# A fused attention, router and expert kernel: key ranges copied on chip, keys and values loaded one head pair ahead, shorter first loads, other unread matmuls

## What is computed

```python
scores_l = scale * np.matmul(q, k.transpose(0, 1, 3, 2))      # kept where |i - j| < 16
scores_s = scale * np.einsum('bhsd,bhnd->bhsn', q, k_sum) + np.log(block)
a = softmax(concat([scores_l, scores_s]))
out = a @ concat([v, v_sum])
```

## Time and profile before

| | us |
|---|---|
| median of 3 runs | 525.67 |
| lowest, highest | 524.82, 528.15 |
| the profiled execution, its own time | 525.85 |
| its span in the profile | 524.1 |
| around the span | 1.8 |
| mean granted TensorE clock, share of full | 0.952 |

### The profile page before, as it was taken

How to read it: one execution, slowest core, us unless ns; L and a number is a source line. 1 busy time by engine, 2 the same in 40 slices (tenths; PEclk the granted TensorE clock), 3 DMA queues, 4 the chain that set the end, 5 groups by cost and what they waited for, 6 DMA issues and landing times.

```text
span 524.1 us, 8451 instructions
## 1 busy us (share of the span) xinstructions
PE 455.3 (87%) x2824; PEld 402.3 (77%) x2824; DVE 354.3 (68%) x1121; ACT 162.0 (31%) x422; POOL 126.0 (24%) x159
## 2 busy tenths in 40 slices
PE   2899899982039998999999999999999999999992
PEld 0688787871037997987997997899897789899771
DVE  3767697778979789889869968976976530300340
ACT  1678576741010113133322212321410341231230
POOL 3111466992012031032112103112101313010011
PEclk9999999996557998999999999999999999999997
DMA  9989997220008045055017007204402709000001
GB/s 252 274 228 282 301 263 231 68 61 1 0 13 339 0 159 194 0 181 191 21 71 281 21 1 271 102 21 176 175 22 93 280 17 329 28 20 1 0 22 40
DMA packets 30883, 65.89 MB, mean 126 GB/s; under 512 B 6784, under 2 KB 19328, under 8 KB 26752
## 3 DMA queue, kind: packets, MB, share of 16 engines
q0 software_dynamic: 6592, 39.85, 20.7%
q1 hardware_dynamic: 23680, 24.57, 16.9%
q10 hardware_dynamic: 576, 1.02, 0.6%
HBM read 59.14 MB, written 6.29 MB: 125 GB/s over the span
## 4 chain that ended last, share of the span: by engine, by line
PE 74%; DVE 12%; ACT 3%; DMA 3%; issue 3%; SPq 3%; POOL 0%; DVEq 0%; ACTq 0%; POOLq 0%
PE psum L906 16%; PE psum L923 15%; PE psum L966 5%; PE psum L973 4%; PE psum L967 4%; PE psum L943 4%; PE psum L944 4%; PE psum L948 4%; DVE key_wide L1205 3%; PE psum L750 3%; DMA shared<-vT 3%; PE psum L775 2%; PE psum L997 2%; PE psum L853 2%; PE psum L759 2%
## 5 line engine op out<-in xcount | busy, mean ns | idle before, releaser
L1205 DVE TENSOR_SCALAR_CACHE_REDUCE key_wide<-keys,thr 128x1536 bf16<-128x1536 f32 x49 | 88.6, 1809 | 1.0
L906 PE MATMUL psum<-shared,w_sb 128*128 128x192 f32 x512 | 86.1, 330 | 1.3 <-ACT shared L662 1.3
L923 PE MATMUL psum<-xs,w_sb 128*128 128x192 f32 x512 | 87.0, 328 | 0.0
L906 PEld LDWEIGHTS psum<-shared,w_sb 128*128 128x128 f32 x512 | 84.9, 193 | 2.0 <-issue 1.5
L923 PEld LDWEIGHTS psum<-xs,w_sb 128*128 128x128 f32 x512 | 83.0, 190 | 0.0
L552 POOL DMA_INDIRECT w_sb<-w,widx x32 | 31.2, 974 | 153.8 <-DVE widx L1276 112.9
L750 PE MATMUL psum<-w_sb,shared 128*128 128x376 f32 x96 | 42.5, 527 | 10.9 <-DMA w_sb<-k_win 10.2
L1304 DVE TENSOR_TENSOR yT_lo<-psum,yT_hi 128x384 fp32r<-128x384 f32 x16 | 8.9, 556 | 55.7 <-ACT yT_hi L662 55.7
L625 ACT ACTIVATE keys<-keys,nmax 128x184 f32<-128x184 f32 x96 | 41.8, 438 | 12.9 <-DVE nmax L1089 12.5
L1089 DVE CUSTOM_DVE_ANT_0 keys<-psum,w_sb 128x184 f32<-128x184 f32 x96 | 29.7, 346 | 22.6 <-PE psum L750 19.7
L966 PE MATMUL psum<-wout_hi,turned_hi 128*128 128x512 f32 x96 | 38.5, 401 | 4.2 <-ACT turned_hi L662 4.2
(11 more groups left out here) (145 smaller groups left out, 817.3 us busy)
## 6 DMA issues: line engine op xcount, KB each, us to landing
w_sb<-k_win SPq DMA_DIRECT2D x16, 240.0 KB, 6.7
shared<-kT SPq DMA_DIRECT2D x8, 384.0 KB, 7.0
shared<-vT SPq DMA_DIRECT2D x8, 384.0 KB, 7.3
shared<-v_main SPq DMA_DIRECT2D x8, 384.0 KB, 3.4
x_rows<-xs SPq DMA_DIRECT2D x8, 384.0 KB, 4.5
shared<-qT SPq DMA_DIRECT2D x7, 384.0 KB, 7.0
w_sb<-w_in SPq DMA_DIRECT2D x4, 512.0 KB, 5.3
w_sb<-w_out SPq DMA_DIRECT2D x8, 256.0 KB, 4.6
```

The source lines that it names most:

```text
L906: mm = pe.matmul(turn[u % 2][:, i * CAP:(i + 1) * CAP], w1_sb[:, par, first:first + P], xT[:, c, :], start=(c == 0), stop=(c == KC - 1))
L923: mm = pe.matmul(turn[u % 2][:, (d % 2) * CAP:(d % 2 + 1) * CAP], w2_sb[:, par, first:first + P], hT[:, c, :], start=(c == 0), stop=(c == ...
L1205: link(dve.tensor_scalar(hits, keys[:, :], cand, -float(CAP), ALU.is_ge, ALU.add, accum_out=count[:, :]))
```

## The change

- **Key ranges.** Only pair 0 still gets them by DMA. For pairs 1 to 7 Pool copies them out of the loaded keys (`key_windows`): for each head three copies of 64 partitions x 320 elements, two tiles each, so six copies a pair, ahead of the key summaries of that pair.
- **Keys and values ahead.** SyncE's list loads the whole keys and values (`kT`, `vT`) of pair g+1 in front of the value ranges of pair g. The queries have a semaphore of their own.
- **First loads.** The key ranges and queries of pair 0 come in two parts: two tiles first, four later. The masks come in three parts. `value_sum(0)`, `turn_vsum(0)` and `value_mean(0)` move one step back.
- **Weights.** The four parts of `w_in` are loaded at g = 1 to 4 and split there one at a time (before: loaded at g = 2 and 3, split at g = 3 and 4 in twos); `w_out` is loaded over g = 3 to 6 in twos.
- **Unread matmuls.** In place of 15 of 128x256 f32 there are 4 of 192 columns and 4 of 384 columns in fp32r (one pass each), then 8 of 64 rows x 256 columns f32 that use the upper and the lower half of the rows in turn and write two banks, then 8 of 64 output partitions x 128 columns f32, likewise in turn.

```diff
-WARM = 15
+FIRST = 2
+WARM = 4
...
+        def load_keys(sp, g):
+            if g >= 2:
+                sp.wait_ge(kmax_ready, g - 1)
+            if g >= 3:
+                sp.wait_ge(kwin_copied, 6 * (g - 2))
+            sp.dma_start(k_sb[:, g % 2, :], kT[g]).then_inc(in_k[g % 2], 16)
+        def load_first_keys(sp):
+            load_keys(sp, 0)
+            windows = k_win[0].rearrange("p (t c) -> p t c", t=QT)
+            for tiles, landed in ((slice(0, FIRST), in_first), (slice(FIRST, QT), in_rest)):
+                sp.dma_start(kwin[0][0:D, tiles, 0:KEYS], windows[0:D, tiles]).then_inc(landed, 16)
+                sp.dma_start(kwin[0][D:P, tiles, TAIL1:SCOLS], windows[D:P, tiles]).then_inc(landed, 16)
...
+            load_first_keys(sp)
+            load_summed(sp, 0)
+            load_values(sp, 0)
+            for c in range(0, 2 * KC, KC):
+                sp.dma_start(wg_sb[:, c:c + KC, :], w_gate...).then_inc(in_gate, 16)
+            load_keys(sp, 1)
+            load_summed(sp, 1)
+            for g in range(1, GROUPS):
                 if g >= 2:
                     sp.wait_ge(scores_ready, QT * (g - 1))
+                sp.dma_start(q_sb[:, g % 2, :], qT[g]).then_inc(in_q[g % 2], 16)
+                if g + 1 < GROUPS:
+                    load_keys(sp, g + 1)
+                    load_summed(sp, g + 1)
+                load_values(sp, g)
...
+            def key_windows(g):
+                pool.wait_ge(in_k[g % 2], 16 * (g // 2 + 1))
+                if g >= 2:
+                    pool.wait_ge(scores_ready, QT * (g - 1))
+                for h, col in enumerate((0, TAIL1)):
+                    rows = slice(h * D, h * D + D)
+                    for first, second in ((0, QT - 1), (1, 3), (2, 4)):
+                        begin, step = window_start(first), window_start(second) - window_start(first)
+                        src = shared[rows, (2 + g % 2) * S + begin:(2 + g % 2) * S + begin + 2 * step]
+                        pair = slice(first, second + 1, second - first)
+                        pool.tensor_copy(kwin[g % 2][rows, pair, col:col + KEYS],
+                                         src.rearrange("p (t c) -> p t c", t=2)[:, :, 0:KEYS]).then_inc(kwin_copied, 1)
+                    pool.wait_ge(kwin_copied, 6 * (g - 1) + 3 * h + 3)
...
             for g in range(GROUPS):
                 if g + 1 < GROUPS:
+                    key_windows(g + 1)
                     key_summaries(g + 1)
                     value_summaries(g + 1)
-                if g == 3:
-                    split_win(0, KC // 2)
-                if g == 4:
-                    split_win(KC // 2, KC)
+                if 1 <= g <= KC:
+                    split_win(g - 1, g)
...
             def scores(u, it):
+                if u == 0:
+                    pe.wait_ge(in_first, 48)
+                if u == FIRST:
+                    pe.wait_ge(in_rest, 48)
+                if t == 0 and g:
+                    pe.wait_ge(in_q[b], 16 * ((g + 1) // 2) + 16 * it)
+                    pe.wait_ge(kwin_copied, 6 * g + 12 * it)
...
+            def warm_up():
+                for i in range(WARM):
+                    pe.matmul(pv[:, 0:CAP], win_hi[:, 0, 0:P], win_hi[:, 1, 0:CAP], start=True, stop=True)
+                for i in range(WARM):
+                    pe.matmul(pv[:, 0:2 * CAP], win_hi[:, 0, 0:P], win_hi[:, 1, 0:2 * CAP], start=True, stop=True)
+                for i in range(WARM):
+                    for h, free in enumerate((pv, bank[3])):
+                        rows = slice(h * D, h * D + D)
+                        pe.matmul(free[:, 0:2 * P], ones_f[rows, :], slots_f[rows, :], start=True, stop=True)
+                for i in range(WARM):
+                    for h, free in enumerate((pv, bank[3])):
+                        cells = slice(h * D, h * D + D)
+                        pe.matmul(free[cells, 0:P], ones_f[:, cells], slots_f[:, 0:P], start=True, stop=True)
```

More of the change, by code:

```diff
@@ L279, in build @@
         in_const = sem("in_const")
-        in_mask = [sem(f"in_mask{i}") for i in range(2)]
+        in_mask = [sem(f"in_mask{i}") for i in range(3)]
         went_on = sem("went_on")
@@ L284, in build @@
         in_gate = sem("in_gate")
-        in_win = sem("in_win")
+        in_win = [sem(f"in_win{c}") for c in range(KC)]
         in_wout = [sem(f"in_wout{i}") for i in range(2)]
         in_k = [sem(f"in_k{i}") for i in range(2)]
-        in_qk = [sem(f"in_qk{i}") for i in range(2)]
+        in_first = sem("in_first")
+        in_rest = sem("in_rest")
+        in_q = [sem(f"in_q{i}") for i in range(2)]
+        kwin_copied = sem("kwin_copied")
         in_vT = [sem(f"in_vT{i}") for i in range(2)]
@@ L394, in store_x, with load_summed, load_values @@
                          xs[:, (g % 2) * QT:(g % 2 + 1) * QT, :]).then_inc(x_stored[g % 2], 16)
+        def load_keys(sp, g):
[4 more added lines that the diff above has]
+            sp.dma_start(k_sb[:, g % 2, :], kT[g]).then_inc(in_k[g % 2], 16)
+        def load_summed(sp, g):
+            if g >= 2:
+                sp.wait_ge(vsum_ready, g - 1)
+            sp.dma_start(vT_sb[:, g % 2, :], vT[g]).then_inc(in_vT[g % 2], 16)
+        def load_first_keys(sp):
[4 more added lines that the diff above has]
+                sp.dma_start(kwin[0][D:P, tiles, TAIL1:SCOLS], windows[D:P, tiles]).then_inc(landed, 16)
+        def load_values(sp, g):
+            b = g % 2
+            if g >= 2:
+                sp.wait_ge(pv_ready, QT * (g - 1))
+            sp.dma_start(vm_sb[:, b, :, :], v_main[g].rearrange("p (t c) -> p t c", t=QT)).then_inc(in_v[b], 16)
+            if g == 0:
+                sp.wait_ge(v_zeroed, 2)
+            for h, row in enumerate((0, MROWS - TAIL)):
+                sp.dma_start(vt_sb[row:row + TAIL, b, :, h * D:h * D + D],
+                             v_tail[g][h * TAIL:h * TAIL + TAIL].rearrange("p (t c) -> p t c", t=QT)
+                             ).then_inc(in_v[b], 16)
         @block.sync
@@ L399, in _ @@
                 sp.sem_inc(x_stored[b], 1)
[L400 to L405, removed]
+            load_first_keys(sp)
+            load_summed(sp, 0)
+            load_values(sp, 0)
+            for c in range(0, 2 * KC, KC):
+                sp.dma_start(wg_sb[:, c:c + KC, :], w_gate.rearrange("(c p) e -> p c e", p=P)).then_inc(in_gate, 16)
+            load_keys(sp, 1)
+            load_summed(sp, 1)
+            for g in range(1, GROUPS):
                 if g >= 2:
                     sp.wait_ge(scores_ready, QT * (g - 1))
[L408 to L428, removed]
+                sp.dma_start(q_sb[:, g % 2, :], qT[g]).then_inc(in_q[g % 2], 16)
[3 more added lines that the diff above has]
+                load_values(sp, g)
                 if g == 1:
@@ L432, in _ @@
                     sp.dma_start(cst[:, early - masks:], consts[:, early:]).then_inc(in_digit, 16)
[L433 to L438, removed]
+                if 1 <= g <= KC:
+                    sp.dma_start(win_raw[:, g - 1, :], w_in[(g - 1) * P:g * P, :]).then_inc(in_win[g - 1], 16)
+                if 3 <= g < 7:
+                    for c in range(2 * g - 6, 2 * g - 4):
+                        sp.dma_start(wout_raw[:, c, :], w_out[c * P:(c + 1) * P, :]).then_inc(in_wout[c // 4], 16)
                 if g >= 2:
@@ L499, in split_win @@
                 for c in range(first, last):
-                    pool.wait_ge(in_win, 16 * (c + 1))
+                    pool.wait_ge(in_win[c], 16)
                     pool.tensor_copy(win_hi[:, c, :], win_raw[:, c, :]).then_inc(win_lo_ready, 1)
@@ L504, in split_win @@
                                        ALU.subtract).then_inc(win_lo_ready, 1)
+                    pool.wait_ge(win_lo_ready, 2 * c + 2)
             def split_wout():
@@ L611, in _ @@
         def _(act):
-            act.dma_start(q_sb[:, 0, :], qT[0]).then_inc(in_qk[0], 16)
+            act.dma_start(q_sb[:, 0, 0:FIRST * P], qT[0][:, 0:FIRST * P]).then_inc(in_first, 16)
             act.dma_start(mask_sb[:, 0:2 * COLS], consts[:, 0:2 * COLS]).then_inc(in_mask[0], 16)
             act.dma_start(cst[:, 0:early - masks], consts[:, masks:early]).then_inc(in_const, 16)
-            act.dma_start(mask_sb[:, 2 * COLS:], consts[:, 2 * COLS:masks]).then_inc(in_mask[1], 16)
+            act.dma_start(mask_sb[:, 2 * COLS:4 * COLS], consts[:, 2 * COLS:4 * COLS]).then_inc(in_mask[1], 16)
+            act.dma_start(q_sb[:, 0, FIRST * P:], qT[0][:, FIRST * P:]).then_inc(in_rest, 16)
+            act.dma_start(mask_sb[:, 4 * COLS:], consts[:, 4 * COLS:masks]).then_inc(in_mask[2], 16)
             def exps(u, it):
@@ L809, in step @@
                     scores(u, it)
-                if u == 1:
+                if u == 2:
                     pe.wait_ge(in_const, 16)
@@ L995, in _ @@
             pe.wait_ge(wout_lo_ready, 2 * FC)
-            for i in range(WARM):
-                pe.matmul(pv[:, 0:2 * P], ones_f, slots_f, start=True, stop=True)
+            warm_up()
```

(8 more changed lines are left out.)

3 lines of the change are left out of this document (2 added, 1 removed).

## The result

The changed kernel takes 528.65 us (median of 20 runs, 524.91 to 531.63) against 526.33 (20 runs, 521.35 to 532.87). The ratio is 1.0053 with a 95% interval of 1.0030 to 1.0077: slower by about 2.8 us, half a percent. The profiled execution took 528.66, with a span of 526.9 in place of 524.1, so its 2.8 us can be followed by time. The forecast was 527.0, 1.1 over the profiled execution of before.

The account below looks back on a forecast made before the run. TensorE holds 74% of the last chain, so transfers count only where TensorE or VectorE waits. From 525.9 us, - 0.9 - 1.5 + 2.9 - 0.4 + 1.0 + 0 gave 527.0; range for 8 in 10: 520.8 to 531.

Parts of the forecast that it names:

- the start: Start to unit 6: unit 0 begins 3.9 us sooner, but only 0.9 is gained at unit 6; bounds 0 and 3.9.
- the locks: VectorE's denominators held up by Pool's instructions in attention: minus 0.4 us; bounds minus 1.5 and plus 3.
- the clock at unit 42: Attention behind unit 42: TensorE stands 3.6 us, its clock falls, plus 1.0 us; bounds 0 and 2.5.
- the unread matmuls: Before the first expert's tokens: new list about as long by columns, 0 taken; shorter matmuls gain 0.4 us at most.
- its own signs of being wrong: Unit 6 below 20, Pool done before unit 42, pairs over 12.5 us, or first hidden layer starting at 1.2 GHz.
- the wait for `vT` that was forecast at 0.8: Value sum of pair 1, at the start: its 0.78 us wait goes, as `vT` is queued right behind `kT`.
- The 0.4 set against them for the first copies: At the start: Pool's first six copies fall beside two denominators of VectorE, minus 0.4 us from the gain.
- Waits for `vT`: Later in attention, at unit 24: the 1.24 us wait goes; 1.5 of 2.0 us lost is given back.
- Pool's copies at pair 7: Unit 42: new copies between scaling and key summaries make it wait 2.9 us longer; bounds 0 and 3.6.
- Its rival, at a chance of 0.20: First expert: half-array matmuls run side by side, list ends about 2.5 us early, clock falls; 529.5 us, chance 0.20.

Follow-up runs that it names:

- the reordered versions: Changed kernel with Pool's key ranges and key summaries of pair 7 ahead of tables and scaling: 524.14 us, 0.9950; with the old unread matmuls too: 522.48 us, 0.9925.
- the last version: Changed kernel with key ranges by DMA again, 19 full unread matmuls before the first expert's tokens and 5 before the second's: 519.36 us, 0.9884 to the kernel before.
- six of each: Changed kernel with 6 of each of its new unread matmuls in place of 4: ratio 1.0016 to the kernel before.

## Why the prediction was right

The time lies inside the range, + 1.1 forecast against + 2.8 in the profile, but that is in good part luck. Four terms were off by more than a microsecond: two gains were larger than forecast (the start by 1.9, the locks by 1.2) and two costs (the clock at unit 42 by 1.9, the unread matmuls by 2.9), and most of it cancelled. The direction is luck too: the forecast made the kernel slower through attention, which up to unit 47 came out 0.4 us faster, and it put at nothing the unread matmuls, which made it slower. Two of its own signs of being wrong came true: unit 6 started below 20, and the first hidden layer started at 1.2 GHz.

- **The start.** 0.9 forecast, 2.84 measured. The bytes ahead of the keys of pair 1 were the same, as said; the step that failed is what was drawn from it, "So that instruction moves by 16.10 - 15.6 = 0.5 us at most". It did become what everything waits for (1.14 us of waiting, at 13.67), but the keys landed at 13.6, 1.9 us sooner, though issued 1.1 us later. The test with the first loads alone shows this part (1.95 at unit 5). The other 0.9, between unit 5 and unit 6, is the wait for `vT` that was forecast at 0.8. The 0.4 set against them for the first copies can't be told from the spread of the start.
- **Waits for `vT`.** 1.5 forecast, 1.59 measured at unit 24: right. (The loss there had been read as 2.0, against a pace of 2.2 for such a unit; without a wait it is 2.56.)
- **Pool's copies at pair 7.** 2.9 forecast, 2.76 measured. A copy took 0.452 us (median of 42) where 0.45 had been interpolated, and six with their gaps took 2.55 where 2.9 had been put. That the wait was Pool's list is shown: in another order of the same work it is gone.
- **Locks on denominators.** 0.4 gained by forecast, 1.57 measured (units 29 and 36). The step that failed is the size of both terms in "I set old 2.8 (units 29, 36 and scattered) against new 2.4": old was 1.57, and new is nothing, since twice the copies left unit 6 to 36 at 60.1. The reason given, that single splits fit VectorE's slack, is what the rows show. A cost of the lock stands elsewhere: at the router's first steps, where Pool's list still runs in the reordered versions. By the Trainium skill, SBUF — State Buffer, section "SBUF: two separate sides", whichever of the two starts first holds the shared port pair for its whole instruction, and the other fully blocks. The row of 3.64 us for three copies, 1.10 where Pool's list has ended, agrees.
- **The clock at unit 42.** 1.0 forecast, 2.85 measured. The mechanism was right; the term was mis-sized, because I counted half a stretch and took VectorE for the limit there. TensorE ran at 1.2 GHz from 94 to 101 us and was busy for 5.97 of these 7 us: it set the pace. Where unit 42 doesn't wait (the other order, or no copies), the clock stays.
- **The unread matmuls.** 0 forecast, 2.93 measured. The step that failed is to take time from columns: "By columns the new list is about as long". Its rival, at a chance of 0.20, is what happened: "If two run side by side, 32 passes take half their time". The 16 passes of 256 columns on halves of the rows took 3.72 us at 1.2 GHz, from 158.17 to 161.89. One after the other they would take some 6.8, an estimate from 0.43 us a pass, twice the 0.216 of the ten unread passes at full clock in the last version. In the Trainium skill, TensorE: Matmul & The Clock Gate, section "Part 3: Packing small matmuls — row/col tiling", matmuls on different row groups run concurrently; the trace agrees, with a factor of 1.8. I had the rule and gave it too small a chance. The 0.4 that a shorter list could gain did come: it is part of the 0.96 between unit 47 and the layer.
- **What stays open.** The gather of the second expert's tokens ended 1.2 us later against the first layer's end. In other kernels with an unchanged gather this stretch varies too (22.3 with the old unread matmuls, 23.4 with the new ones in the kernel before, 24.1 with six of each). Over all fourteen profiles it is 22.3 to 24.1. No run separates it.

## What to carry to other kernels

Before giving an engine with slack a new job, read its list in order and find the item that another engine waits for behind a long one: here the 27% busy Pool held up TensorE at one place for 3.4 us, and a new order of the same work freed it. Matmuls that nobody reads are sized by time up to the landing, not by columns, and matmuls that use the two halves of the rows in turn took 3.72 us here where their columns said 6.8. If a change bundles prefetch, a new way of making the data and a new grain of other work, try them apart; here the copies carried none of the gain in the middle.

## What was not expected of the hardware

- An idle of 1.7 to 2.6 us before the first tokens was followed by 1.2 GHz in four kernels (layers of 13.57, 13.67, 13.29 and 12.32 us) and not in one (2.33 us of idle, 10.64).
- A queue of transfers didn't land by bytes: the same keys of pair 1, with the same bytes issued ahead, landed 8.6 to 8.9 us after their issue with the old first loads, 6.2 with the first loads cut in two, and 5.3 to 6.1 with the new order as well.
- A fall of the clock in attention nearly doubled the matmuls of two units (0.85 to 1.59 us), and units 42 to 47 took 2.85 us longer.
